# Retention and mixture-of-experts kernel: indirect transfers tied to the experts' chunks, first weight splits and buffer fills moved

## What is computed

```python
scores = scale * np.matmul(q, k.transpose(0, 1, 3, 2))
Dmat = np.where(rel >= 0, gamma[:, None, None] ** rel[None, :, :], 0.0)
attn = np.matmul(scores * Dmat, v)                 # -> x: 2304 rows of 512
logits = x @ w_gate
expert_idx = np.argmax(logits, axis=1)             # gate_w: softmax at that expert
...                                                # disp[e, slot] = x[i], in order of i
h = np.maximum(np.einsum('ecd,edf->ecf', disp, w1), 0.0)
y = np.einsum('ecf,efd->ecd', h, w2)
out[i] = gate_w[i] * y[expert_idx[i], pos[i]]      # capacity 576 rows per expert
```

## Time and profile before

| what | us |
|---|---|
| median of three runs | 442.7 |
| lowest, highest | 439.44, 444.29 |
| the profiled execution's own time | 443.09 |
| its span (first to last instruction) | 441.1 |
| PE busy | 385.3 (87% of the span) |
| DVE, ACT, POOL busy | 219.4, 185.4, 133.3 |

### The profile page before, as it was taken

How to read it: one execution, slowest core, us unless ns; L and a number is a source line. 1 busy time by engine, 2 the same in 40 slices (tenths; PEclk the granted TensorE clock), 3 DMA queues, 4 the chain that set the end, 5 groups by cost and what they waited for, 6 DMA issues and landing times.

```text
span 441.1 us, 10744 instructions
## 1 busy us (share of the span) xinstructions
PE 385.3 (87%) x3553; PEld 354.4 (80%) x3554; DVE 219.4 (50%) x445; ACT 185.4 (42%) x367; POOL 133.3 (30%) x131
## 2 busy tenths in 40 slices
PE   7889999989988799769788997997998799899990
PEld 3879899879953699759778995996998799898980
DVE  2144665772772476246416552752754465654730
ACT  1243434323410365245325453643654455554730
POOL 1532344465203610620160036017006204204012
PEclk9997999986996999889988999999799599999997
DMA  8887988766898345424433443544444344452001
GB/s 270 236 272 236 328 241 248 210 201 194 280 312 257 107 158 162 137 96 145 169 111 115 143 143 116 190 146 131 165 144 142 125 163 143 135 172 78 7 0 47
DMA packets 26858, 73.60 MB, mean 167 GB/s; under 512 B 7050, under 2 KB 7178, under 8 KB 26704
## 3 DMA queue, kind: packets, MB, share of 16 engines
q1 hardware_dynamic: 20432, 63.77, 44.8%
q0 software_dynamic: 6400, 9.46, 7.0%
HBM read 64.81 MB, written 19.92 MB: 192 GB/s over the span
## 4 chain that ended last, share of the span: by engine, by line
PE 74%; issue 7%; DVE 6%; DMA 5%; another core or an unknown queue 3%; ACT 2%; SPq 1%; POOL 1%; POOLq 0%; ACTq 0%; DVEq 0%
PE bank L571 17%; PE bank L573 16%; PE bank L572 15%; PE bank L427 4%; PE bank L451 4%; PE bank L559 3%; PE bank L441 3%; PE bank L477 3%; PE bank L470 3%; PE bank L564 2%; PE bank L459 2%; DMA q_dec<-in_qdecay 2%; DMA qk_raw<-in_qk 2%; DVE at_slot L867 1%
## 5 line engine op out<-in xcount | busy, mean ns | idle before, releaser
L571 PE MATMUL bank<-m_hi,w_hi 128*128 x512 | 160.4, 313 | 15.3 <-ACT y_nat L694 8.2
L573 PE MATMUL bank<-m_lo,w_hi 128*128 x512 | 156.8, 306 | 5.8 <-issue 5.7
L572 PE MATMUL bank<-m_hi,w_lo 128*128 x512 | 157.5, 308 | 1.9 <-issue 1.9
L571 PEld LDWEIGHTS bank<-m_hi,w_hi 128*128 128x128 f32 x512 | 100.0, 195 | 23.9 <-issue 22.1
L776 DVE TENSOR_TENSOR w_lo<-w_raw,w_hi 128x512 fp32r<-128x512 f32 x128 | 89.9, 704 | 38.5 <-ACT w_hi L651 38.3
L572 PEld LDWEIGHTS bank<-m_hi,w_lo 128*128 128x128 f32 x512 | 100.4, 196 | 3.6 <-issue 3.4
L573 PEld LDWEIGHTS bank<-m_lo,w_hi 128*128 128x128 f32 x512 | 99.9, 195 | 3.7 <-issue 3.7
L368 POOL DMA_INDIRECT out<-y_nat,slot_row x40 | 42.6, 1066 | 197.7 <-ACTq L757 179.1
L651 ACT ACTIVATE w_hi<-w_raw 128x512 fp32r<-128x512 f32 x128 | 80.2, 628 | 25.0 <-PE bank L573 24.9
L953 DVE SCALAR_TENSOR_TENSOR m_lo<-bank,m_hi 128x384 fp32r<-128x384 f32 x64 | 35.5, 555 | 74.5 <-ACT m_hi L733 51.4
L733 ACT ACTIVATE m_hi<-bank 128x384 fp32r<-128x384 f32 x64 | 31.5, 492 | 75.5 <-PE bank L573 38.8
(11 more groups left out here) (87 smaller groups left out, 370.0 us busy)
## 6 DMA issues: line engine op xcount, KB each, us to landing
w_raw<-in_moe_w SPq DMA_DIRECT2D x64, 512.0 KB, 3.3
qk_raw<-in_qk SPq DMA_DIRECT2D x24, 384.0 KB, 3.8
kv_raw<-in_kv SPq DMA_DIRECT2D x24, 384.0 KB, 4.9
x_rows<-x_nat SPq DMA_DIRECT2D x24, 192.0 KB, 4.5
out<-zeros SPq DMA_DIRECT2D x12, 384.0 KB, 4.7
q_dec<-in_qdecay SPq DMA_DIRECT2D x1, 1152.0 KB, 8.0
out<-y_nat,slot_row POOLq DMA_INDIRECT x40
x_gat<-x_rows,slot_row POOLq DMA_INDIRECT x37
```

The source lines that it names most:

```text
L571: pe.matmul(dst, w_hi[:, s, i, :], hi[:, i, cols], start=(i == 0), stop=False)
L572: pe.matmul(dst, w_lo[:, s, i, :], hi[:, i, cols], start=False, stop=False)
L573: last = pe.matmul(dst, w_hi[:, s, i, :], lo[:, i, cols], start=False, stop=(i == K4 - 1))
```

## The change

Three edits move things, and one splits a warm-up.

1. POOL's indirect DMAs in the experts' stage wait, besides for what they waited for, for the product of one chunk each (`after_chunk`): for expert e the three a scatters for chunks 1 to 3, the two b scatters for 4 and 5, the three a gathers for 6 to 8, the two b gathers for 9 and 10. The releases of `y_nat` and `b_y_nat` move with them: the first to the start of the expert, the second behind the b scatters. Before the loop, the two b gathers of expert 0 wait for the first two `xs_lo_made`. After the last expert the a scatters now go ahead of the b scatters.
2. The first four weight splits leave the first batch: `w_high` goes to ACT's end of the routing, `w_low` to DVE's, behind the instruction that sets `routed`.
3. POOL's three fills go from the last batch to the first, behind chunks 2, 3 and 4; `cast_tables` goes from chunk 2 to chunk 4; POOL waits for the table `q_dec` only ahead of a `qs`, no longer ahead of the first `k_sc`.
4. Of PE's three warm-up blocks before the first scores one goes behind them.

```diff
@@ gpsimd
-            pool.wait_ge(q_dec_in, 16)
                 if c > 0:
+                    wait(pool, q_dec_in, 16)
                     pool.wait_ge(qk_in[c % 3], 16 * (2 * b + c // 3 + 1))
...
-                    if last and c < 3:
-                        pool.memset((x_gat, y_sb, y_nat)[c][:, :, :], 0.0).then_inc(zero_made, 1)
+                    if first and 1 < c < 5:
+                        pool.memset((x_gat, y_sb, y_nat)[c - 2][:, :, :], 0.0).then_inc(zero_made, 1)
...
             for g in range(NA, NG):
+                pool.wait_ge(xs_lo_made, NA + g - NA + 1)
                 gather(0, g)
             pool.wait_ge(out_zeroed, 16 * ZERO_STEPS)
+            def after_chunk(e, j):
+                if e < E:
+                    pool.wait_ge(result_made, e * CHUNKS + j + 1)
             for e in range(E + 1):
+                for g in range(NA):
+                    wait(pool, scattered[g], 16 * (e - 1))
+                pool.sem_inc(y_nat_free, 1)
                 if e > 0:
+                    for g in range(NA):
+                        pool.wait_ge(y_scaled, NA * (e - 1) + g + 1 + SCALED0)
+                        after_chunk(e, g)
+                        scatter(e - 1, g)
                     for g in range(NA, NG):
                         pool.wait_ge(b_y_scaled, NB * (e - 1) + g - NA + 1)
+                        after_chunk(e, g)
                         scatter(e - 1, g)
-                for g in range(NA):
-                    wait(pool, scattered[g], 16 * (e - 1))
-                pool.sem_inc(y_nat_free, 1)
+                for g in range(NA, NG):
+                    wait(pool, scattered[g], 16 * e)
+                pool.sem_inc(b_y_nat_free, 1)
                 if e + 2 < E:
...
+                        after_chunk(e, NG + g)
                         gather(e + 2, g)
                 if e + 1 < E:
...
+                        after_chunk(e, NG + g)
                         gather(e + 1, g)
-                if e > 0:
-                    for g in range(NA):
-                        pool.wait_ge(y_scaled, NA * (e - 1) + g + 1 + SCALED0)
-                        scatter(e - 1, g)
-                for g in range(NA, NG):
-                    wait(pool, scattered[g], 16 * e)
-                pool.sem_inc(b_y_nat_free, 1)
@@ tensor
-            keep_warm(3)
+            keep_warm(2)
             pe.wait_ge(scores_cleared, 1)
             scores(0, 0)
+            keep_warm(1)
@@ scalar
-                    if first and 1 < c < 4:
-                        w_high(0, 2 * c - 4)
-                        w_high(0, 2 * c - 3)
...
             act.activation(l_exp[:, :, :], l_dif[:, :, :], ACT.Exp).then_inc(exp_made, 1)
+            for j in range(SLOTS):
+                w_high(0, j)
@@ vector
-                    if first and c == 2:
+                    if first and c == 4:
                         cast_tables()
-                    if first and 1 < c < 4:
-                        w_low(0, 2 * c - 4)
-                        w_low(0, 2 * c - 3)
...
             dve.tensor_tensor(slot_gate[:, :, 1:1 + E], map_sb[:, :, 3, :], gate_a[:, :, :], ALU.add).then_inc(routed, 1)
+            for j in range(SLOTS):
+                w_low(0, j)
```

8 lines of the change are left out of this document (4 added, 4 removed).

## The result

The changed kernel takes 408.98 us (median of four runs, 403.87 to 410.14), the kernel before beside it 441.47 (four runs, 439.44 to 444.29): a ratio of 0.922 with a 95% interval of 0.911 to 0.933. The forecast was 403.5 us, range 395 to 424.

What follows compares the result with a forecast made beforehand. It took the kernel to be bound by ACT's ReLU waiting for PE increments held late during POOL's bursts of indirect DMAs. Sum: 443.1 - 32 - 5 - 5 + 2.6 = 403.7 us profiled, forecast 403.5, range 395 to 424.

Steps and rivals of the forecast that it cites:

- The spread: Experts' stage: POOL's transfers placed behind single chunks end the late increments; 32 us gained, bounds 0 and 34.9.
- PE's increment arrives late as long as POOL's burst runs, and comes when the burst is over: Experts' stage: explanation of ACT's ReLU waits, 36.6 us in eight waits; the burst rows' loss is 34.9 us.
- another cause: Rival, experts' stage: the remote wait has its own cause whatever POOL does; 34.9 us remain, 435.7 us; chance 0.04.
- The loss starts after some five or six in a row: POOL's bursts in the experts: loss not proportional to transfers; ten lose 5.6 to 8.4 us, seven lose 1.8.
- Start and fills: Before the experts: earlier start gains 5 us (bounds 0 and 5.8), moved POOL fills 5 us (bounds 1.8 and 6.9).
- The splits in the tail: Behind the routing: four w_high and four w_lo cost 0; SP's loads behind them 0, bounds -1 and +1.
- The end: After the last expert: two b scatters behind the a scatters cost 1.29 us each; 2.6 us lost.
- Half: Rival, experts' stage: single or bunched transfers still hold increments; gain 17 instead of 32, 418.7 us; chance 0.18.
- hold by number: Rival, experts' stage: the hold follows the number of transfers, not their density; 34.9 us stay, 435.7 us; chance 0.07.
- Slower: Rival, ACT's ReLU in chunks 1 to 10: every transfer holds the next increment; 447.7 us at 0.7 each; chance 0.04.
- experts 1 to 5 shorter by 5.6 to 8.4 us each: Sign in the profile after, experts' stage, that the spread removes each expert's loss.
- a first gather that lands later behind the splits: Sign of being wrong, at POOL's first gathers, where the moved splits were priced at 0.

Runs made afterwards that it cites:

- spread_only: The kernel before with only the changed kernel's POOL block of the experts' stage; 419.13 us against 441.18.
- late_burst: The changed kernel with an expert's ten indirect DMAs back to back behind the seventh product; 428.99 us, one run.
- start_only: The kernel before with only the changed start (POOL's later wait for q_dec, PE's moved warm-up block); 408.2 us against 408.05.
- sets 2 and 3: Two groups of four follow-up kernels, each run beside the kernel before (404.08 and 408.05 us), none with a late increment.
- end_order: The changed kernel with the last expert's two b scatters ahead of its a scatters again; 400.76 us, ratio 1.000 to the kernel before.
- two_fives: The changed kernel with an expert's ten transfers in two bursts of five, behind chunks 3 and 8; 403.86 us, ratio 0.990 to the kernel before.
- moves_only: The changed kernel with the kernel before's POOL block, so start, fills and splits alone; 431.57 us, ratio 0.982 to the kernel before.
- no_b: The kernel before without the b transfers of all experts; 415.2 us, ratio 0.940 to the kernel before.
- fills_back: The changed kernel with POOL's three fills in the last batch again; 410.33 us, ratio 1.017 to the kernel before.
- splits_back: The changed kernel with the first four weight splits in the first batch again; 403.92 us, ratio 1.011 to the kernel before.
- best: The changed kernel with splits back in the first batch, last b scatters first, b_y_nat released behind the gathers; 400.54 us, ratio 0.984 to the kernel before.
- loads_later: The changed kernel with SP loading the second expert's weights only after expert 0's first three turned groups; 408.74 us, ratio 1.028 to the kernel before.

## Why the prediction was right, and where not

**The spread: forecast 32 us gained, measured 32.1.** The reading of place was right: POOL's run of transfers, PE's late increments, and ACT waiting for them (spread_only and late_burst). The size was right for these executions. The step that was incomplete is "PE's increment arrives late as long as POOL's burst runs, and comes when the burst is over". The runs showed in its place: it may, in some sets of runs, and even there some get through during the burst (the one at 338.18 us above). In the others the same bursts cost nothing, and the term is 0. That the comparison fell in a set of the first kind was luck, as far as the forecast goes: nothing in it said that the 32 us could be absent. I estimate the changed kernel without the hold at 408.3 - (248.5 - 242.8) = 402.6 us, and the kernel before at 443.1 - (280.6 - 242.8) = 405.3, with the experts' stage of start_only; the change itself was not run in sets 2 and 3. Its nearest relatives there have ratios of 1.000 (end_order, with a shorter end) and 0.990 (two_fives).

The forecast's argument against "another cause" was that ACT's wait ends 1.5 us after the burst. That showed the burst to be one condition. It could not show it to be the only one, and one profiled execution never can. The Trainium skill (DMA: Bandwidth & Descriptors, section "Anatomy of one DMA — SWDGE (gpsimd) path") has it that many descriptors can be emitted before their cost shows. The trace of start_only agrees (ten in a row, clock 1.00, no late increment), those of the kernel before and of moves_only do not.

**The length of a run.** "The loss starts after some five or six in a row" rested on experts 5 and 6 in the earlier trace rows. The changed kernel's bunches of five still cost 0.9 to 1.4 us in each of experts 0 to 5, and no_b's cost 0 to 4.6. As a guide to spread further it was good, as a number it wasn't. The forecast kept back 2.9 us for it (34.9 less 32); it is 7.6 us of excess less the 1.5 of start_only, 6.1. What there was to lose was larger as well, 38.6 less 1.5, 37.1 us instead of 34.9. The two errors, 3.2 and 2.2 us, offset each other for the most part, the other 1.1 us of the stage lie outside the sixteen products, and that the term came out to 0.1 us is luck. Five gathers bunch, too, where the prediction allowed for two or three.

**Start and fills: forecast 10 us, measured 8.5.** The four kernels without both moves end the retention stage at 124.1 to 128.4 us, the seven with all of them at 114.3 to 119.6, on average 126.6 and 117.4: 9.1 us. The split was off: the start was to bring 5 and brought 1.5 (start_only). POOL's first `k_sc` did move, from 11.69 to 7.19 us:

```profile
7.19 1.03 POOL L351 TENSOR_TENSOR k_sc<-kv_raw,const 96x512 f32<-96x512 f32 x1 [4.62 <-DMA kv_raw<-in_kv]
```

but the stage hardly got shorter by it. The loads seem to set its pace, which no run here shows by itself: the DMA engines are 89% busy over the changed kernel's retention stage, and were 80%. For the fills the row is plain; the longest `at_slot` is 1296 ns, not 3464:

```profile
L878 DVE TENSOR_SCALAR at_slot<-const,pos x24: 475/509/1296, 56.1 to 124.0; 96x576 bf16<-96x576 f32 x24
```

while start_only, with the fills in the old place, has 3680 again. What the parts do apart isn't settled to a microsecond: taking back the splits or the fills alone left the stage at 115.3 and 116.7 us, and the time at half clock ahead of its end ranges from 3.4 us (fills_back) to 30.7 (no_b), which is 2 to 15 us of time. As a rough estimate, take half of the time at half clock off each stage. Without the moves it is then 117.0, 117.9 and 117.3 us (before, spread_only, start_only) and 113.0 (no_b), with all of them 110.3 to 113.7. Splits_back has 111.9 and best 112.7, fills_back 115.0. By this estimate the fills carry most of the gain and the splits' place next to nothing; with 113.0 in no_b it is a hint and not a proof.

**The splits in the tail: forecast 0 with bounds -1 and +1, measured +2.1.** This is the step that failed. Six executions without this move take 9.0 to 10.2 us from the first gather to the first `x_gat` turn, on average 9.6; seven with it 10.9 to 14.2, on average 12.3. The splits themselves cost little, though not nothing: the first gather takes 1.62 us, and 1.21 in the kernel before and in splits_back.

```profile
129.45 1.62 POOL L362 DMA_INDIRECT y_nat<-x_rows,slot_row  x1 [17.42 <-DVE slot_row L949]
131.38 1.01 POOL L362 DMA_INDIRECT y_nat<-x_rows,slot_row  x1 [0.31 <-issue]
```

The longer first gather goes with the splits in all fourteen profiles: 1.62 to 1.63 us in the eight with them in the tail, loads_later among them, and 1.20 to 1.21 in the six without. The Trainium skill (SBUF — State Buffer, section "Who interferes with whom") says that a DVE instruction with two inputs in SBUF, as `w_lo` is, contends with a GpSimd instruction that reads SBUF. The same section of the Trainium skill adds, marked as inferred, that making DMA descriptors needs the write side of what DVE and GpSimd share, and that this kind of instruction takes the read side only. The 0.4 us would fit the first; the earlier trace rows had shown a gather of 1.00 beside a `w_lo`, so by what mechanism the splits lengthen the first gather stays open. The larger part is SP's two loads of 512 KB each, which wait for these splits and start with the gathers. In loads_later, where only they are moved, the 9.2 us are back. The prediction named these loads and priced them without a row; the DMA queue's share beside the first gathers would have been the thing to ask.

**The end: forecast +2.6, measured +3.8.** The last scatter, to be held against the earlier trace rows:

```profile
397.35 0.98 POOL L368 DMA_INDIRECT out<-y_nat,slot_row  x1 [0.30 <-issue]
```

From the last product to the last scatter it is 433.27 - 427.7 = 5.6 before and 397.35 - 389.2 = 8.2 after, the 2.6 of two transfers. The other 1.2 us are the time from there to the program's end, which was taken as constant. end_order gave the 3.8 back.

**The sum.** Forecast 403.7 for the profiled execution, measured 408.3. The 4.6 are 1.5 (retention stage), 2.1 (loads beside the first gathers) and 1.2 (the drain), less 0.1 of the spread and rounding.

**The rivals.** "Half" and "hold by number" are refuted for this comparison by the experts' stage. "Slower" had single transfers holding increments in every chunk; chunks 1 to 9 of the changed kernel follow each other at the median distance. "Another cause" was given 0.04, and is the one that came back: not instead of the burst, but as a second condition beside it. Of the prediction's signs, "experts 1 to 5 shorter by 5.6 to 8.4 us each" was met by two of five: their excess fell by 4.5, 4.7, 4.9, 6.4 and 7.4 us. The sign of being wrong "a first gather that lands later behind the splits" did come.

## What to carry to other kernels

A wait "remote" beside a burst of one engine shows that the two coincide, not that the burst alone suffices. Before spending a redesign on it, run the old kernel again on another occasion: here it gave back 33 us with no edit. And count what a trace lacks before reading a record's absence as an event. Spreading transfers over the work that they accompany is still a sound precaution, as the experts' stage is no longer for it where there is no hold (243 us with bursts and without), and 22 us of the median were saved by it alone where there was.

When work moves, list what waits for it on the other queues. The four splits were nearly free where they went (0.4 us on the first gather); the two loads that they release were not. And order what stands at the very end by what must land last: two transfers in the wrong place cost 3.8 us, not the 2.6 of their issue.

## What the runs showed of the hardware that was not expected

Increments by PE can reach a waiting ACT up to 9.5 us after the matmul that makes them, while POOL issues indirect DMAs back to back and ACT's own increments reach DVE within 0.11 us, and on another occasion on the same chip the same program text in that stage has none of 128 later than 0.02 us. POOL's own pace doesn't tell the two apart: its transfers follow each other at no less than 1.28 to 1.29 us in all fourteen profiles, with a median of 1.00 to 1.01 us each. What the second condition is stays open. One thing in the traces goes with it: where increments are late, records of increments are missing, 12 to 26% of those by DMAs in the six executions with late increments, and under 1% in the eight without. Whether the missing records and the late increments have one cause, and whether the hold would be there with no recording at all, no run here tells: each execution of this document has its span and granted clock on record, so some recording ran in all of them. The rest was found to be the same: the median matmul, ACTIVATE and fill have the same durations, and in the stretch in which the earlier trace rows waits no instruction code was being loaded. To repeat the kernel before and the changed one side by side without late increments, and best with them, would be the next runs.
